# Sparse attention and routed experts on one core: the last group's order, and late routing in bfloat16 parts

## What is computed

```python
scores = scale * q @ k.T                          # 4 batches, 8 heads, 576 rows, head size 64
kth    = np.partition(scores, -32)[..., -32]      # 32nd largest of each row
scores = np.where(scores >= kth, scores, -1e9)
attn   = softmax(scores);  x = attn @ v           # x: 4 x 576 tokens of 512
logits = x @ w_gate;  local = sigmoid(x @ w_local)
e[s]   = argmax(logits[s]) if s == 0 or local[s] < 0.5 else e[s-1]   # per batch, in sequence
out[s] = softmax(logits[s])[e[s]] * (relu(x[s] @ w1[e[s]]) @ w2[e[s]])
```

## Time and profile before

| | |
|---|---|
| median of 3 runs | 1034.29 us |
| lowest and highest | 1033.83 and 1036.27 us |
| the profiled execution | 1033.68 us |
| its span | 1031.70 us |
| mean granted clock of PE in it | 0.838 |
| busy: PE, DVE, ACT, POOL | 799.3, 762.4, 417.0, 612.9 us |

### The profile page before, as it was taken

The page is one execution under the profiler, slowest core; times in us unless marked ns, Lnnn a source line. Parts: engine busy times, 40 slices in busy tenths (PEclk is TensorE's granted clock), DMA queues, the critical chain, the costliest instruction groups (busy, mean ns, idle before and its releaser), DMA issues. The chain is left out here.

```text
span 1031.7 us, 15965 instructions
## 1 busy us (share of the span) xinstructions
PE 799.3 (77%) x3928; PEld 454.6 (44%) x3929; DVE 762.4 (74%) x1617; ACT 417.0 (40%) x913; POOL 612.9 (59%) x557
## 2 busy tenths in 40 slices
PE   2566757666766665579989989989746999999996
PEld 1343434443433343345555555545434444444442
DVE  5999999999999998999999999899833111111010
ACT  2445554555545455235555665655520111111110
POOL 0877888788878887478888888798501011111111
PEclk7677686767668687568999999999955999999998
DMA  3091101010010103010541545354400045453610
GB/s 119 1 372 35 49 1 49 14 35 17 31 47 0 47 13 127 14 55 9 223 168 75 221 184 187 111 194 174 174 24 30 21 168 231 175 201 135 240 32 27
DMA packets 17498, 103.96 MB, mean 101 GB/s; under 512 B 2638, under 2 KB 5198, under 8 KB 13328
## 3 DMA queue, kind: packets, MB, share of 16 engines
q1 hardware_dynamic: 10560, 57.68, 15.0%
q10 hardware_dynamic: 3024, 34.19, 8.5%
q0 software_dynamic: 3840, 11.28, 3.1%
HBM read 93.70 MB, written 10.75 MB: 101 GB/s over the span
## 5 line engine op out<-in xcount | busy, mean ns | idle before, releaser
L1194 POOL TENSOR_SCALAR p_sb<-s_sb,top 128x576 f32<-128x576 f32 x141 | 313.7, 2225 | 98.3 <-DVE top L917 95.3
L917 DVE MAX8 top<-work 128x8 f32<-128x576 f32 x432 | 307.0, 808 | 0.0
L395 PE MATMUL ps<-id_sb,p_sb 128*128 128x128 f32 x720 | 130.2, 322 | 180.3 <-ACT p_sb L723 180.3
L925 DVE MATCH_REPLACE8 work<-top,work 128x576 f32<-128x576 f32 x288 | 216.8, 806 | 0.0
L1197 POOL TENSOR_TENSOR p_sb<-p_sb,s_sb 128x576 f32<-128x576 f32 x141 | 198.8, 1410 | 25.9 <-POOL p_sb L1194 23.5
L395 PEld LDWEIGHTS ps<-id_sb,p_sb 128*128 128x128 f32 x720 | 96.3, 165 | 227.9 <-issue 227.9
L1098 DVE TENSOR_SCALAR moe<-ps 128x512 f32<-128x512 f32 x30 | 20.8, 692 | 193.4 <-PE ps L645 193.4
L385 PE MATMUL ps<-qk_sb 64*128 64x288 f32 (+1 forms) x640 | 139.1, 575 | 6.8 <-DMA qk_sb<-in_qk 5.9
L731 ACT ACTIVATE pT_sb<-ps 128x640 f32<-128x640 f32 x144 | 101.3, 703 | 104.1 <-PE ps L395 102.9
L723 ACT ACTIVATE p_sb<-p_sb,nmax 128x576 f32<-128x576 f32 x144 | 110.8, 770 | 76.9 <-POOL p_sb L1197 76.6
L424 PE MATMUL ps<-pT_sb,v_sb 128*64 128x64 f32 (+5 forms) x1152 | 126.2, 383 | 10.3 <-ACT pT_sb L731 10.0
(11 more groups left out here) (140 smaller groups left out, 728.6 us busy)
## 6 DMA issues: line engine op xcount, KB each, us to landing
w_sb<-in_w SPq DMA_DIRECT2D x16, 2048.0 KB, 10.0
w_sb<-in_w ACTq DMA_DIRECT2D x16, 2048.0 KB, 10.7
qk_sb<-in_qk SPq DMA_DIRECT2D x16, 864.0 KB, 4.6
v_sb<-in_v SPq DMA_DIRECT2D x16, 320.0 KB, 2.9
x_dram<-x_sb SPq DMA_DIRECT2D x2, 1024.0 KB, 5.9
x_dram<-x_sb SPq DMA_DIRECT2D x2, 768.0 KB, 4.6
x_dram<-x_sb SPq DMA_DIRECT2D x2, 256.0 KB, 2.4
wg_sb<-in_wg ACTq DMA_DIRECT2D x1, 292.0 KB, 8.0
```

The source lines that it names most:

```text
L395: mm = pe.transpose(ps[:, 2 + c // 4, (c % 4) * P:(c % 4 + 1) * P], p_at(n % GROUP)[:, c * P:(c + 1) * P], id_sb[:, :])
L917: dve.max(top[:, par, j, rnd, :], src).then_inc(chain, 1)
L925: dve.match_replace(work[:, j, :], top[:, par, j, rnd, :], src, NEG).then_inc(chain, 1)
L1194: pool.tensor_scalar(p_at(j)[:, 0:S], s_at(n % RING), top[:, k % 2, j, ROUNDS - 1, 7:8], -BIG, ALU.is_lt, ALU.mult).then_inc(masked, 1)
```

## The change

**Last group.** The loop of PE and ACT now stops before k = 5 of the last step, which is written out: PE turns the first tile of k = 5 ahead of values(4), the second one into banks 0 and 1 (which the scores no longer use), the third into banks 2 and 3, where it waits only for the turn two before it. ACT does the three exponentials first. The last `add_logits` waits for the first of the three activations behind the copy of the logits, where it waited for all three.

**Choice.** In the late routing, keep is one operation where it was two. `carry` and `code` go to PE as two tensors. `carry` comes back through ACT into SBUF, and the scan reads `code`'s rows from PSUM; L1038 and L1039 are gone. `weigh` stands behind the counts.

**Rows.** The tile number is now a rounding (adding and taking off 1.5 * 2^23). One-hots are bfloat16, and so is what they are multiplied with: a token number is split into a multiple of 64 and a remainder, a gate into three bfloat16 parts. The 18 products of PE are bfloat16 and carry tokens alone; a second set of 18 for the gates, 78 columns wide, stands behind the first `turn_rows`, and ahead of the first expert's products. The gates' operations on DVE stand behind the row numbers.

```diff
+            def turn(r, n, bank=2, slots=1):
                 t = 2 * TPU * r + n
-                hold(pe, pT_done, BIAS + t)
+                hold(pe, pT_done, BIAS + t - slots + 1)
...
-                for k in range(GROUPS):
+                for k in range(GROUPS - last):
...
-            values(UNITS // 2 - 1, GROUPS - 1, range(GROUP - 1))
-            values(UNITS // 2 - 1, GROUPS - 1, range(GROUP - 1, GROUP))
-            turn_back(UNITS // 2 - 1, GROUPS - 1)
+            r, k = UNITS // 2 - 1, GROUPS - 1
+            turn(r, GROUP * k)
+            values(r, k - 1)
+            pe.wait_ge(evac, BIAS + TILES)
+            turn(r, GROUP * k + 1, 0, 2)
+            turn(r, GROUP * k + 2, 2, 2)
+            turn_back(r, k - 1)
+            values(r, k, range(GROUP - 1))
+            values(r, k, range(GROUP - 1, GROUP))
+            turn_back(r, k)
             pe.wait_ge(code_ready, 2)
             for b in range(2, B):
-                mm = code_rows(b, 0, TPU)
+                mm = code_rows(b, 0, TPU, carry)
+            mm.then_inc(carry_ps, 1)
+            for b in range(2, B):
+                mm = code_rows(b, 2, TPU)
             mm.then_inc(code_ps, 1)
...
-                mm = pe.matmul(ps[:, 7, 0:2 * NTA], lane_of[:, c, :], marks[:, c, :], start=c == 0, stop=c == COLS - 1)
+                mm = pe.matmul(ps[:, 7, 0:2 * NTA], lane_of[:, c, :], token_marks[:, c, :], start=c == 0,
+                               stop=c == COLS - 1)
             mm.then_inc(rows_ps, 1)
...
             turn_rows(0, 0, 0)
+            pe.wait_ge(gates_ready, 1)
+            for c in range(COLS):
+                mm = pe.matmul(ps[:, 6, 0:3 * NTA], lane_of[:, c, :], gate_marks[:, c, :], start=c == 0,
+                               stop=c == COLS - 1)
+            mm.then_inc(gates_ps, 1)
...
+            r, k = UNITS // 2 - 1, GROUPS - 1
+            for j in range(GROUP):
+                exponentiate(r, GROUP * k + j)
+            take_pT(r, GROUP * k)
+            take_oT(r, k - 1)
+            take_pT(r, GROUP * k + 1, 0)
+            take_pT(r, GROUP * k + 2)
+            normalise(r, k - 1)
+            take_oT(r, k)
+            normalise(r, k)
+            act.wait_ge(carry_ps, 1)
+            act.activation(s_sb[2 * 32:P, S:2 * S], ps[2 * 32:P, 0:2, :].rearrange("p b n -> p (b n)")[:, 0:S],
+                           ACT.Copy).then_inc(carry_done, 1)
...
-                step(dve.tensor_scalar(keep[:, c], lg[:, c, E], -1.5 * 2.0 ** -23, None, ALU.is_gt))
-                step(dve.tensor_tensor(keep[:, c], keep[:, c], may_keep[:, c], ALU.mult))
-                dve.tensor_tensor(code[:, c], keep[:, c], fresh[:, c], ALU.max).then_inc(code_ready, 1)
+                step(dve.scalar_tensor_tensor(out=keep[:, c], in0=lg[:, c, E], scalar=-1.5 * 2.0 ** -23, in1=may_keep[:, c],
+                                              op0=ALU.is_gt, op1=ALU.mult))
+                if late:
+                    dve.tensor_copy(carry[:, c], keep[:, c])
+                    dve.scalar_tensor_tensor(out=code[:, c], in0=keep[:, c], scalar=0.5, in1=fresh[:, c],
+                                             op0=ALU.is_lt, op1=ALU.mult).then_inc(code_ready, 1)
...
-            step(dve.tensor_scalar(carried, codes, float(2 * E), None, ALU.is_ge))
-            step(dve.scalar_tensor_tensor(out=fresh_row, in0=carried, scalar=0.5, in1=codes, op0=ALU.is_lt, op1=ALU.mult))
+            dve.wait_ge(carry_done, 1)
             step(dve.tensor_tensor_scan(placed, carried, fresh_row, 0.0, ALU.mult, ALU.add))
...
+            step(dve.tensor_scalar(slot[:, :], place[:, :, E], -(P + 1) / 2.0, 1.0 / P, ALU.add, ALU.mult))
+            step(dve.tensor_scalar(tile_of[:, :], slot[:, :], ROUNDER, -ROUNDER, ALU.add, ALU.add))
+            step(dve.tensor_tensor(at_tile[:, :, :], by_tile(tile_of[:, :]),
+                                   tiles_of[:, 0:NTA].unsqueeze(1).to_broadcast([P, COLS, NTA]), ALU.is_equal))
+            dve.sem_inc(tiled, 1)
+            step(dve.scalar_tensor_tensor(out=lane[:, :], in0=tile_of[:, :], scalar=-float(P), in1=place[:, :, E],
+                                          op0=ALU.mult, op1=ALU.add))
+            dve.tensor_tensor(token_marks[:, :, 0:NTA], at_tile[:, :, :], by_tile(tok_sb[:, 1, :]),
+                              ALU.mult).then_inc(high_ready, 1)
...
             step(dve.tensor_scalar(row_f[:, :], ps[:, 7, 0:NTA], float(SKIP), None, ALU.add))
+            step(dve.tensor_tensor(row_f[:, :], row_f[:, :], ps[:, 7, NTA:2 * NTA], ALU.add))
...
+            for n in range(3):
+                mark = dve.tensor_tensor(gate_marks[:, :, n * NTA:(n + 1) * NTA], at_tile[:, :, :],
+                                         by_tile(gate_bits[:, n, :]), ALU.mult)
+            mark.then_inc(gates_ready, 1)
             rows(0, 0, 0)
+            dve.wait_ge(gates_ps, 1)
...
-            for k in range(2):
-                add_logits(UNITS // 2 - 1, GROUPS - 2 + k)
+            add_logits(UNITS // 2 - 1, GROUPS - 2)
+            add_logits(UNITS // 2 - 1, GROUPS - 1, 1)
             pool.wait_ge(tiled, 1)
-            pool.tensor_tensor(named, gated, tok_sb[:, :].unsqueeze(2).to_broadcast([P, COLS, NTA]),
-                               ALU.mult).then_inc(named_ready, 1)
+            pool.tensor_tensor(token_marks[:, :, NTA:2 * NTA], at_tile[:, :, :],
+                               tok_sb[:, 2, :].unsqueeze(2).to_broadcast([P, COLS, NTA]), ALU.mult).then_inc(low_ready, 1)
```

More of the change, by code:

```diff
@@ L108, in build @@
         code = sb("code", [P, COLS], BF16)
+        carry = sb("carry", [P, COLS], BF16)
         idb_sb = sb("idb_sb", [P, P], BF16)
@@ L116, in build @@
         slot = sb("slot", [P, COLS])
-        lane = sb("lane", [P, COLS])
+        lane = sb("lane", [P, COLS], BF16)
+        lanes = sb("lanes", [P, P], BF16)
         tile_of = sb("tile_of", [P, COLS])
         gate = sb("gate", [P, COLS])
-        tok_sb = sb("tok_sb", [P, COLS])
+        tok_sb = sb("tok_sb", [P, 3, COLS])
+        at_tile = sb("at_tile", [P, COLS, NTA], BF16)
+        token_marks = sb("token_marks", [P, COLS, 2 * NTA], BF16)
+        gate_marks = sb("gate_marks", [P, COLS, 3 * NTA], BF16)
+        lane_of = sb("lane_of", [P, COLS, P], BF16)
+        gate_bits = sb("gate_bits", [P, 3, COLS], BF16)
+        gate_rest = sb("gate_rest", [P, COLS])
         base_sb = sb("base_sb", [P, 1])
@@ L184, in build @@
         at += COLS
-        lanes = small_sb[:, at:at + P]
+        lane_row = small_sb[:, at:at + P]
         def full_tiles(x, j):
@@ L807, in ahead @@
                         take(r + 1, n - 2 * TPU)
-                for k in range(GROUPS):
-                    final = last and k == GROUPS - 1
+                for k in range(GROUPS - last):
                     ahead(k, 0)
@@ L821, in step @@
                     exponentiate(r, GROUP * k + 2)
-                    if not final and (k > 0 or not first):
+                    if k > 0 or not first:
                         normalise(*before(r, k))
@@ L1030, in _ @@
             late = slice(TPU, COLS)
-            choose(late)
-            weigh(late, 2)
+            choose(late, True)
             high = slice(2 * 32, P)
-            carried, fresh_row, placed = (s_sb[high, n * S:(n + 1) * S] for n in range(3))
-            codes = ps[high, 0:2, :].rearrange("p b n -> p (b n)")[:, 0:S]
+            placed, carried = s_sb[high, 0:S], s_sb[high, S:2 * S]
+            fresh_row = ps[high, 2:4, :].rearrange("p b n -> p (b n)")[:, 0:S]
             dve.wait_ge(code_ps, 1)
-            step(dve.tensor_scalar(carried, codes, float(2 * E), None, ALU.is_ge))
-            step(dve.scalar_tensor_tensor(out=fresh_row, in0=carried, scalar=0.5, in1=codes, op0=ALU.is_lt, op1=ALU.mult))
+            dve.wait_ge(carry_done, 1)
             step(dve.tensor_tensor_scan(placed, carried, fresh_row, 0.0, ALU.mult, ALU.add))
@@ L1048, in _ @@
                               accum_out=ntile[:, 0:1]).then_inc(ntile_ready, 1)
+            weigh(late, 2)
             dve.wait_ge(counts_ps, 1)
@@ L1060, in by_tile @@
                 return x.unsqueeze(2).to_broadcast([P, COLS, n])
[L1062 to L1072, removed]
+            step(dve.tensor_scalar(slot[:, :], place[:, :, E], -(P + 1) / 2.0, 1.0 / P, ALU.add, ALU.mult))
[7 more added lines that the diff above has]
+                              ALU.mult).then_inc(high_ready, 1)
             for c in range(0, COLS, LANES):
-                dve.tensor_tensor(lane_of[:, c:c + LANES, :], lanes.unsqueeze(1).to_broadcast([P, LANES, P]),
+                dve.tensor_tensor(lane_of[:, c:c + LANES, :], lanes[:, :].unsqueeze(1).to_broadcast([P, LANES, P]),
                                   lane[:, c:c + LANES].unsqueeze(2).to_broadcast([P, LANES, P]),
@@ L1103, in _ @@
             rows(0, 0, 0)
+            dve.wait_ge(gates_ps, 1)
+            step(dve.tensor_copy(row_gate[:, :], ps[:, 6, 0:NTA]))
+            for n in range(1, 3):
```

(6 more changed lines are left out.)

68 lines of the change are left out of this document (37 added, 31 removed).

## The result

The changed kernel takes 1019.79 us (median of 4 runs, 1018.5 to 1021.58), beside 1034.06 for the kernel before (4 runs). Ratios further down are to the kernel before as timed beside that run. The ratio is 0.986, 95% interval 0.9838 to 0.9882. The forecast was 1021.5, range 1018 to 1026.5. The profiled execution took 1019.15 with a span of 1017.3.

What follows compares the result with a forecast made beforehand. Attention was taken as bound by its VectorE search, then a one-engine-at-a-time sequence delays TensorE's expert products, which run to the end. Terms sum to 12.8 us off 1033.7, 1020.9; with the median 0.6 above, 1021.5, range 1018 to 1026.5.

Steps and rivals of the forecast that it cites:

- The last group: Reordered turns and values of the last attention group, up to the end of values(5): -5.2 us (2.3 to 5.6).
- the 2.8 that I took: Duration in us assumed for values(4) in the last group, 3.29 before, as part may be at full clock.
- One sign that the forecast had named as wrong: Turns of 1.3 us in the last group, listed among what would show the forecast wrong.
- the ends 1.9 and 5.2: Last group's gain in us with everything at half clock, 1.9, and with the clock mostly full, 5.2.
- The rival with half clock throughout: TensorE at half clock through the last group: gain there only 2.3, experts perhaps 1 us longer, total 1025.4; chance 0.17.
- The choice: Late routing, from the choice (L944) to the scan, 4.87 us before: -1.7 us.
- The tile number: Late routing, from slot to the first lane piece, 4.27 us before: -1.6 us (1.5 to 2.4).
- Lanes and rows: From the first lane piece to the row numbers, 8.62 us before, 3.6 expected: -5.0 us (4.6 to 5.1).
- the rival with 0.08: Lane pieces run at double rate on DVE, about 0.28 us instead of 0.48; total 1020.5; chance 0.08.
- The gates: 18 gate products on PE ahead of the first expert product, 2.0 us less 1.3 of wait: +0.7 us (-1.5 to +4).
- one more operation: An added operation of 26 elements before the row numbers: +0.2 us.
- an operation less on DVE: Early routing loses one small operation on DVE, which is the bound there: -0.2 us (0 to 0.4).

Runs made afterwards that it cites:

- seven kernels: The changed kernel and those with edits on the remainder, float32 marks, the gates and the choice, all with the same last-group lines; mask to choice 14.70 to 15.69 us.
- The two experiments on the remainder's product: Changed kernel with POOL's product for the token number's remainder made by ACT (median 1018.18 us), or as a second DVE operation (one run, 1020.69 us).

## Why the prediction was right

**The last group** (forecast 5.2, measured 5.23; shown by taking the order out, 5.5, and by putting it in alone, 4.2, which come to 4.8 to 5.0 without the slow turn ahead of them). Step by step: exponential at 740.72 and turn at 741.72, 1.00 apart as read. values(4) took 3.47, worse than the 2.8 that I took, wholly at half clock; values(5) took the 1.97 of the earlier trace rows, at full. One sign that the forecast had named as wrong did come, a turn of 1.3 in the last group: the first took 1.30 (which the sum itself had allowed for), the two after it 1.85 together. I had set 4.8 for the order between the ends 1.9 and 5.2, and it gave 4.8: from the last values' end less the shift of the mask, 756.28 - 750.73 - 0.73. The rival with half clock throughout did not come, but a part of its cost did. That the stretch agrees to 0.03 is luck: the same lines gave 14.70 to 15.69 in seven kernels, by where the clock fell and rose, so the forecast is confirmed to about 1 us.

**The choice** (1.7; 1.77). ACT's copy took the 0.65 worked out between 0.49 and 0.70. The scan from PSUM took 1.36, like the 1.35 of the earlier trace rows. Of the 1.77 the second tensor and `weigh` behind the counts gave 1.4, keep in one operation 0.2, and 0.2 is the gap that closed without a reason found. The cover for `weigh` held: L1088 starts 0.6 after the end of its last operation (L1001, 761.52 and 0.23, in the timeline of DVE).

**The tile number** (1.6; 1.66). This was the term where row and plan parted. L1067's 0.48 was read as POOL and DVE excluding each other, and the term lowered by 0.8 for it. The two experiments on the remainder's product show it: 1.26 beside POOL, 0.65 beside ACT, and no gain against DVE alone. The forecast had 1.5 for the 1.26. The Trainium skill's rule ("SBUF — State Buffer", section on the two separate sides), exclusive for the whole instruction and whoever starts first, agrees: POOL started at 766.99 and DVE at 767.21.

**Lanes and rows** (5.0; 5.33). The right engine was named for each side of it. The size of a bfloat16 product was a guess, 0.11, half the float32 pitch. Three take 0.31 including the last result, where I had put 0.33 and 0.3 in sum: 0.3 too much. That the lane pieces would run at double rate was the rival with 0.08; they take 2.89 in bfloat16 and 2.89 in float32. (By its own working, 0.17 fixed and half of the remainder, that rival's piece is 0.33 and not 0.28, and DVE's gain 0.9 and not 1.2.) The tier table of the Trainium skill ("VectorE: DVE Perf Modes") gives tensor_tensor in bfloat16 twice the rate, and the pieces did not get it. The Trainium skill ("Vector Engine (DVE) Microarchitecture Reference", section 5.1) gives the single rate for a two-source operation on 2-byte operands of which one repeats an element, tried there with 16 repeats; here it is 128, and the 2.89 agrees.

**The gates** (0.7 and 0.2 for one more operation; 0.47). 18 products took 1.38, not 2.0, and PE's wait of 1.30 ahead of the first expert product became 0.34. By the starts, 0.26 of the 0.47 lies ahead of the turn (4.34 before, 4.60 after: the one operation more, and the gather) and 0.21 between the turn and the first expert product (2.39 and 2.60). So the term of 0.7 for the products was three times too large, as the size of one was guessed.

**What was missed.** By the span the sum is 1.6 short. 0.3 is in lanes and rows, 0.4 in the gates and 0.1 in the small remainders of the other rows. 0.5 more than forecast stands ahead of the last group, where 0.73 was measured and 0.2 forecast for an operation less on DVE. Neither is shown. In the twelve executions of this study the first mask falls between 737.73 and 740.01, though the kernels are all but equal up to there. The remaining 0.2 is in the experts, where the same instructions took from 236.63 to 238.71: in two things, the first twelve records of expert products (6.09 to 7.55) and a wait of PE for weights (1.02 ending at 961.63 before, 0.87 ending at 946.86 after, and 0 to 0.74 in others). A single execution cannot tell 0.5 us in either place, and the 0.7 that they give beyond the forecast belongs to no part of the change that I could show.

## What to carry to other kernels

In a sequence over several engines with nothing beside it, add starts. Where TensorE's clock has no part, a difference between two starts repeats to a few hundredths from kernel to kernel (scan to slot 8.90 in nine, the same 2.60 or 2.61 from slot to the first lane piece in six), while totals wander by 2 to 3 us; parts of 1 us are to be judged there in the timeline and not by the time. Where the clock rises or falls inside the stretch, a single execution tells less: mask to choice wandered by 1 us with the same lines, choice to scan by 0.25. When an operation of 18 elements takes 0.48 where its like took 0.17 or 0.18, look at what the other engine was doing. Splitting two products between DVE and POOL gained nothing here, while ACT, which was idle, took one off the path. A place given to an unhurried part (the gates) is best where the engine waits for somebody else anyway.

## What the runs showed that I had not expected

Choice to scan took 3.10 in some kernels and 2.85 in others with the same operations (2.95 in one): eight records of PE's code products took 0.69 where the granted clock was half, and seven took 0.41 where it was full. DVE's work split with POOL took as long as DVE alone (2.61 and 2.55). How fast the last turn of k = 4 runs, 0.74 or 1.30, moves all behind it by 0.6, though nothing was changed in it. The 36 float32 passes have a pitch of 0.21 with 52 columns and with 78. A first expert stretch of twelve records varied between 6.09 and 7.55 us with nothing changed in it: in the changed kernel the granted clock there was half for a part, and where it rises differs from execution to execution. Whether the gate products ahead of it make it rise sooner stays open: 6.09 to 7.44 with them, 6.83 without them, 7.14 and 7.55 in the two kernels of the old routing.
